# Two streams of 64-row matmuls in place of 128-row ones, and activations kept in SBUF

## The reference

```
w   = softmax of weight_gen over its 7 taps
x1  = for each token and each of 8 heads of 24 features: sum over the 7 last tokens of w[tap] * x
h1  = x1 @ moe_w_in        (192 -> 2048);   g1 = maximum(0.01 * h1, h1)
x2  = g1 @ moe_w_out       (2048 -> 192)
h2  = x2 @ moe2_w_in       (192 -> 2048);   g2 = where(h2 > 0, h2, exp(minimum(h2, 0)) - 1)
out = g2 @ moe2_w_out      (2048 -> 192)
```

## Time and profile before

| | us |
|---|---|
| median of 3 runs | 1212.63 (1212.58 to 1213.23) |
| profiled execution | 1211.23 |
| its span in the trace | 1209.4 |
| TensorE matmuls busy | 1185.8 (98%) |
| VectorE busy | 814.8 (67%) |
| ScalarE busy | 746.2 (62%) |
| GpSimd busy | 355.1 (29%) |

### The profile page before, as it was taken

The page is one execution under the profiler, slowest core; times in us unless marked ns, Lnnn a source line. Parts: engine busy times, 40 slices in busy tenths (PEclk is TensorE's granted clock), DMA queues, the critical chain, the costliest instruction groups (busy, mean ns, idle before and its releaser), DMA issues.

```text
span 1209.4 us, 14562 instructions
## 1 busy us (share of the span) xinstructions
PE 1185.8 (98%) x5208; PEld 973.0 (80%) x5208; DVE 814.8 (67%) x778; ACT 746.2 (62%) x815; POOL 355.1 (29%) x216
## 2 busy tenths in 40 slices
PE   7798999999999999999999999999999999999998
PEld 5586888888888888888888888888888888888887
DVE  7877775766767666675766767666676766766555
ACT  3365757666575665757666575665756656575675
POOL 5725060240704206061250704307061250700000
PEclk9999999999999999999999999999999999999999
DMA  7231112011110211112010110211112010100001
GB/s 194 61 98 37 27 40 64 26 49 26 51 51 26 66 35 49 26 39 62 26 49 26 47 54 26 63 39 49 26 39 62 26 49 26 39 26 27 14 17 36
DMA packets 44642, 54.24 MB, mean 45 GB/s; under 512 B 4116, under 2 KB 32914, under 8 KB 44624
## 3 DMA queue, kind: packets, MB, share of 16 engines
q1 hardware_dynamic: 44624, 54.01, 14.7%
HBM read 36.29 MB, written 17.69 MB: 45 GB/s over the span
## 4 chain that ended last, share of the span: by engine, by line
PE 92%; DVE 5%; ACT 1%; DMA 0%; POOL 0%; issue 0%; SPq 0%; POOLq 0%; ACTq 0%
PE hidden L516 46%; PE y_b L545 9%; PE y_b L546 9%; PE y_a L552 9%; PE y_a L551 9%; PE y_a L550 9%; DVE hid_lo L952 1%; DVE hidden L913 1%; ACT hid_hi L810 1%; DVE up_b_lo L832 1%; DVE up_a_lo L832 1%; DMA xw<-in_x_dram 0%; PE turn L585 0%; DVE dn L345 0%; PE turn L589 0%; DVE dn L344 0%
## 5 line engine op out<-in xcount | busy, mean ns | idle before, releaser
L952 DVE TENSOR_TENSOR hid_lo<-hidden,hid_hi 128x1024 fp32r<-128x1024 f32 x254 | 311.0, 1225 | 242.0 <-ACT hid_hi L810 242.0
L810 ACT ACTIVATE hid_hi<-hidden 128x1024 fp32r<-128x1024 f32 x254 | 260.8, 1027 | 329.3 <-DVE hidden L913 200.8
L284 POOL TENSOR_TENSOR mix<-xw,wk 128x768 f32<-128x768 f32 x15 | 23.3, 1554 | 684.8 <-DVE wk L859 681.8
L916 DVE SCALAR_TENSOR_TENSOR hidden<-act,hidden 128x1024 f32<-128x1024 f32 x129 | 157.5, 1221 | 98.7 <-ACT act L785 96.7
L516 PE MATMUL hidden<-in_a_hi,up_a_hi 128*128 128x512 f32 x510 | 200.8, 394 | 12.2 <-DVE hid_lo L952 11.6
L545 PE MATMUL y_b<-hid_hi,dn 128*128 128x512 f32 x512 | 199.5, 390 | 1.2 <-DVE dn L345 1.2
L546 PE MATMUL y_b<-hid_lo,dn 128*128 128x512 f32 x512 | 199.3, 389 | 0.0
L552 PE MATMUL y_a<-hid_lo,dn 128*128 128x512 f32 x512 | 199.2, 389 | 0.0
L550 PE MATMUL y_a<-hid_hi,dn 128*128 128x512 f32 x512 | 199.2, 389 | 0.0
L551 PE MATMUL y_a<-hid_hi,dn 128*128 128x512 f32 x512 | 199.2, 389 | 0.0
L516 PE MATMUL hidden<-in_b,up_b_lo 128*128 128x512 f32 x510 | 199.0, 390 | 0.0
(11 more groups left out here) (100 smaller groups left out, 1140.9 us busy)
## 6 DMA issues: line engine op xcount, KB each, us to landing
xw<-in_x_dram SPq DMA_DIRECT2D x14, 960.0 KB
raw_b<-squares_out SPq DMA_DIRECT2D x60, 96.0 KB, 2.2
out_dram<-staged SPq DMA_DIRECT2D x15, 384.0 KB, 2.4
squares_in<-prod SPq DMA_DIRECT2D x56, 96.0 KB, 2.0
squares_out<-ya SPq DMA_DIRECT2D x15, 256.0 KB, 2.0
raw_a<-squares_in SPq DMA_DIRECT2D x14, 256.0 KB, 2.8
raw_d<-in_moe_w_out_dram SPq DMA_DIRECT2D x8, 384.0 KB, 6.2
raw_a<-in_moe_w_in_dram SPq DMA_DIRECT2D x8, 256.0 KB, 4.9
```

The source lines that it names most:

```text
L284: ops.tensor_tensor(dst, src, w, ALU.mult).then_inc(done, 1)
L810: nc.scalar.activation(hid_hi[:, s % 2, :], hidden[:, s % 2, :], ACT.Copy).then_inc(s_hi, 1)
L916: nc.vector.scalar_tensor_tensor(out=h, in0=a, scalar=-1.0, in1=h, op0=ALU.add, op1=ALU.max).then_inc(done, 1)
L952: nc.vector.tensor_tensor(hid_lo[:, s % 2, :], h, hid_hi[:, s % 2, :].bitcast(f32), ALU.subtract).then_inc(s_lo, 1)
```

## The change

Every steady matmul is cut to 64 of the 128 rows: one works on partitions 0 to 63 (LOW), the next on 64 to 127 (HIGH), and they alternate, each stream with its own PSUM bank at a time. What filled 64 of 128 rows twice is now packed closer: `up_b_lo` holds only the lower half of its columns on each half of the rows, and `up_pair` does both halves of a step in one pair, with a second copy of the input `in_b_up` on the upper rows. So a step has 19 pairs in place of 20 matmuls. `y_a` has two banks, one for each stream, which are added at the end (`add_y`). `up` is split into a first and a second half, and `down` into `down_open` and `down_close`; each half of `up` fills one bank from the LOW rows and the other from the HIGH rows, and the second half crosses over.

The nonlinearity writes into `act` in SBUF instead of `hidden`, and `hid_hi` and `hid_lo` read it there. So the first half of `up` waits for the nonlinearity of two steps before (`s_g`), and `down_open` for its `hid_lo`. `take_y` and `add_y` move ahead of the step's own work in step 1. In step 1, `down_close` stands ahead of the second half of `up`.

```diff
         def up(m, src, g, s, second):
+                if not second:
+                    for n in range(3):
+                        up_a(LOW, 0, n)
+                        up_a(HIGH, 1, n)
+                    up_b(LOW, 0)
+                    up_b(HIGH, 1)
+                    up_pair(m, src, s)[1].then_inc(s_open, 1)
+                    return
+                pe.wait_ge(s_open, g)
+                for n in range(3):
+                    up_a(LOW, 1, n)
+                    up_a(HIGH, 0, n)
+                half1 = up_b(LOW, 1, stop=True)
+                half0 = up_b(HIGH, 0, stop=True)
...
+            def up_pair(m, src, s, stop=False):
+                cols = slice(s * P, (s + 1) * P)
+                low = nc.tensor.matmul(hidden[:, s % 2, HALF[0]], up_b_lo[m][LOW, cols], in_b[src][LOW, :], start=False, stop=stop)
+                high = nc.tensor.matmul(hidden[:, s % 2, HALF[1]], up_b_lo[m][HIGH, cols], in_b_up[src][HIGH, :], start=False, stop=stop)
+                return low, high
...
+            def down_close(m, s, d):
+                down_a(m, s, LOW, 0, 1)
+                down_a(m, s, HIGH, 1, 2)
+                down_a(m, s, LOW, 0, 2)
+                pe.wait_ge(s_yblow, d + 1)
+                down_b(m, s, HIGH, 0, 0)
+                down_a(m, s, LOW, 1, 0)
...
             def phase(m, c, ph, dm, dc):
-                        pe.wait_ge(s_lo, g - 1)
-                    up(m, input_of(m, c), g, s)
+                        pe.wait_ge(s_g, g - 1)
+                    up(m, input_of(m, c), g, s, False)
...
+                    pe.wait_ge(s_lo, g - 1)
+                    of, step = (dm, ST - 2 + s) if s < 2 else (m, s - 2)
+                    down_open(of, step, g - 2, ph if s == 2 and dm is not None else None)
+                    if s == 1:
+                        down_close(of, step, g - 2)
+                        up(m, input_of(m, c), g, s, True)
                     else:
+                        up(m, input_of(m, c), g, s, True)
+                        down_close(of, step, g - 2)
...
# ScalarE
+                    nc.scalar.activation(in_b_up[input_of(1, c)][D2:P, :], yb[0][:, :], ACT.Copy)
                     nc.scalar.activation(in_b[input_of(1, c)][0:D2, :], yb[0][:, :], ACT.Copy).then_inc(s_mhi, 1)
...
+                    if s == 1 and dm is not None:
+                        take_y(dm, dc, ph - 1)
                     act_e.wait_ge(s_up, g + 1)
-                        act_e.wait_ge(s_g, g - 1)
+                        act_e.wait_ge(s_lo, g - 1)
-                    if s == 1 and dm is not None:
-                        take_y(dm, dc, ph - 1)
...
-                    nc.scalar.activation(hid_hi[:, s % 2, :], hidden[:, s % 2, :], ACT.Copy).then_inc(s_hi, 1)
+                    nc.scalar.activation(hid_hi[:, s % 2, :], act[:, s % 2, :], ACT.Copy).then_inc(s_hi, 1)
# VectorE
-                    nc.vector.tensor_tensor(h, h, a, ALU.max).then_inc(done, 1)
+                    nc.vector.tensor_tensor(a, h, a, ALU.max).then_inc(done, 1)
...
-                    nc.vector.tensor_tensor(hid_lo[:, s % 2, :], h, hid_hi[:, s % 2, :].bitcast(f32), ALU.subtract).then_inc(s_lo, 1)
+                    nc.vector.tensor_tensor(hid_lo[:, s % 2, :], act[:, s % 2, :], hid_hi[:, s % 2, :].bitcast(f32), ALU.subtract).then_inc(s_lo, 1)
```

More of the change, by code:

```diff
@@ L548, in down_a @@
[L548 to L559, removed]
+                low, high = up_pair(0, input_of(0, 0), 0, stop=True)
@@ new lines, in up_first, with down_b, down_a @@
+                low.then_inc(s_up1, 1)
+                high.then_inc(s_up, 1)
+            def down_b(m, s, rows, i, n):
+                f = 2 * s + i
+                v = (hid_hi, hid_lo)[n]
+                start, stop = f == 0 and n == 0 and rows == LOW, f == FT - 1 and n == 1 and rows == HIGH
+                return nc.tensor.matmul(y_b[:, :], dn[m][rows, f, P:2 * P], v[rows, s % 2, HALF[i]], start=start, stop=stop)
+            def down_a(m, s, rows, i, n):
+                f = 2 * s + i
+                first, v = ((0, hid_hi), (2 * P, hid_hi), (0, hid_lo))[n]
+                bank = y_a[0] if rows == LOW else y_a[1]
+                return nc.tensor.matmul(bank[:, :], dn[m][rows, f, first:first + P], v[rows, s % 2, HALF[i]],
+                                        start=(f == 0 and n == 0), stop=(f == FT - 1 and n == 2))
@@ L561, in down_last @@
             def down_last():
                 s = ST - 1
[L564 to L570, removed]
-                last.then_inc(s_dn, 1)
+                wait_half(pe, s_lo, s_lo1, END, 0)
@@ L584, in sum_first_mix @@
                     for j in range(J):
-                        last = nc.tensor.matmul(turn_cols[:, 0, j], term[:, j, 0:P], ident[:, :], start=False, stop=(end and j == J - 1))
+                        last = nc.tensor.matmul(by_token(turn_a)[:, j], term[:, j, 0:P], ident[:, :], start=False, stop=(end and j == J - 1))
                     if end:
@@ L588, in sum_first_mix, with transpose_mix @@
                     for j in range(J):
[L589 removed]
+                        last = nc.tensor.matmul(by_token(turn_b)[:, j], term[:, j, P:D], ident[:, :], start=False, stop=(end and j == J - 1))
                     last.then_inc(s_mixt if end else s_termu, 1)
[L592 removed]
+            def transpose_mix(c, part):
                 pe.wait_ge(s_mix, c + 1)
[L596 removed]
+                pe.wait_ge(s_xin, 2 * c + part)
+                first, last_col = (0, P) if part == 0 else (P, D)
                 for j in range(J):
[L598 to L600 removed]
+                    last = nc.tensor.transpose(by_token(transposed(c)[part])[:, j], mix[:, j, first:last_col], ident[:, :])
                 last.then_inc(s_mixt, 1)
```

213 lines of the change are left out of this document (138 added, 75 removed).

## The result

The changed kernel takes 1263.41 us (median, 1260.8 to 1265.63) against 1212.76: ratio 1.0416, interval [1.0398, 1.0433]. It is slower by 50.7 us; the forecast was slower by 28.4. The profiled execution is the slowest of its four (1265.63), so the spans of the two profiles are 54.4 us apart.

A forecast was written before the change was run, and what follows sets the result against it. TensorE, busy 98% of the span, was taken as the bound. A chunk of 74.7 us, +2.0, gave +26 over 13 chunks; start +6 and end -2.5 made +29.5 on 1211.23: 1241 us, range 1196 to 1290.

The forecast's parts named there:

- the likeliest case: Whole kernel: the forecast of 1241 us, own range 1226 to 1262, chance 0.63.
- A pair in one slot: TensorE's steady steps: two 64-row matmuls take one slot of 0.2267 us, so a step is 4.31 us, a chunk 68.9.
- MLP 2, 2.6 a chunk: Shorter distances: stall 0.6 in MLP 2, ScalarE's pace 0.2, 1.8 at the next MLP 1 pass; 2.6 us a chunk.
- Lock, 3.1 a chunk: MLP 1 passes: VectorE's `hid_lo` from SBUF and GpSimd's mixing exclude each other, stalling TensorE 3.1 us a chunk.
- The layout: Hand-laid VectorE and GpSimd timeline of an MLP 1 pass: stalls of 2.8 us at step 5, 0.3 at step 6.
- A chunk of 74.7: Steady chunk: 68.9 + 2.6 + 3.1, with 0.1 more, 74.7 us; +2.0 on 72.66.
- Start, +6 (0 to 12): First 120 us: more `hid_lo` waits (+4) and costs of the first passes add 6 us, range 0 to 12.
- End, -2.5: Last passes: no mixing (-1.8), last two MLP 2 passes -1.0 each, work behind the last matmul +1.3; -2.5 us.
- slow pairs: Rival: a pair takes longer than a slot, 0.248 us giving 1300 us, 0.27 about 1370; chance 0.15.
- The lock does not bite: Rival: `hid_lo` and mixing miss each other, a chunk of 71.6, about 1195 us; chance 0.17.

The follow-up runs named there:

- GpSimd only writing: GpSimd's mixing products and additions of chunks 1 to 15 replaced by instructions that only write: 1194.21 us on the kernel before, 1190.63 on the changed kernel.
- the mended order with activations in SBUF: Changed kernel, activations left in SBUF, with `up`'s second half after two pairs of `down` and `take_y` behind the step's own work: 1249.92 us, ratio 1.0315.

## Why the prediction was right, and where it was short

*Sign, mechanism and places: right.* The time lies in the range, 22 us above the forecast and 1 above the likeliest case's own range. The mechanisms are those that the prediction named; the size of the start was not.

- *A pair in one slot*: right, 0.227.
- *MLP 2, 2.6 a chunk*: measured 0.59 in step 3 and 1.84 at the start of MLP 1's pass, with ScalarE's loop at 4.36. Right to 0.1 each. The copies to `in_b_up` cost nothing, as the row at 612.54 shows. That `ylow` and `ya` ahead of Relu(1) cost nothing agrees with these waits, but was not measured by itself.
- *Lock, 3.1 a chunk*: 0.77 for `hid_lo` of step 4, 0.18, and 1.77 for that of step 5, together 2.7. The layout had put 2.8 on step 5 and 0.3 behind it: step 4 was late already. Size right.
- *A chunk of 74.7*: measured 75.33. Long waits are 5.2 (forecast 5.5), 0.6 more lie in slots of 0.33 behind them (not foreseen), and all that is no wait is 69.5 (69.2). Two of the twelve chunks are 1.5 longer, see the last section. Together 12 x 0.6 + 3 = 10 us over the forecast.
- *Start, +6 (0 to 12)*: this is the term that was mis-sized: +15.2 at the third `ylow`, of which 3 are there when the mixing of chunk 1 starts, at 32.16. Two of those 3 are no work of the change: the first product of the program waits for the arrival of `x` until 10.13 in this profile and until 8.17 in that of before; before's own matmuls with SBUF placement had it at 9.8 as well.

```profile
10.13 2.09 POOL L317 TENSOR_TENSOR prod<-xw,wk 128x192 f32<-128x192 f32 x2 [7.39 <-DMA xw<-in_x_dram]
```

  The step that failed is "idle TensorE, made by VectorE's weight splits beside mixing; there fewer slots help little, five more `hid_lo` wait (+4)". The runs show that the whole of that idle time is the lock (GpSimd only writing takes 16.8 us from before's start), so it was no fixed cost with five waits beside it. Each part of the change makes it longer by itself: the third `ylow` comes 6.5 us later with the SBUF placement alone and 9.1 with pairs and the new order alone, but only 2.6 with all of it and GpSimd only writing on both sides. (Less what the arrival of `x` differs by, these are about 4.8, 8.5 and 2.3, and the 15.2 is 13.2.) So splits and `hid_lo` take turns with mixing instructions, and TensorE, which has no work stored up there and shorter distances than before, passes much of it on; then it works at the lower clock for a few us.
- *End, -2.5*: with one chunk's +2.0 that makes -0.5, measured +4.2. The copy, two additions and transposes behind the last matmul were right: 2.38 us from it to the transposes against 1.14. Missing were the waits of the last steps (1.04 at 1251.66, where no `up` is left for TensorE to work on while `hid_lo` is made) and the wait of 1.74 at the last MLP 1 pass.
- *Slips in the sums*: the sum ends at 1241 for the profiled execution, and the 1.4 us by which the median lies above it were named but not added. The window of the earlier trace rows is 25 to 145, not the first 120 us. Outside 13 chunks of 16 steps lie 48 of the 256 steps, not 56, which takes 1.4 us from the 1300 of "slow pairs". The 0.248 of "slow pairs" is two loads, 220, and twice 14; from the columns it would be 0.241. None of these moves the forecast by more than 1.4 us.

*The rivals.* "The lock does not bite" is excluded by the length of `hid_lo` and by the run without it, which at 1190.6 came near to its 1195. "Slow pairs" is excluded by 0.227. The Trainium skill's rule in *SBUF — State Buffer*, "Who interferes with whom", held in every run: `hid_lo` has means of 1371 to 1452 ns where it reads two SBUF operands beside mixing, and of 1223 to 1225 from PSUM or beside mere writes. Of *TensorE: Matmul & The Clock Gate*, Part 3, the near-simultaneous start of row groups is what the records show, and two groups run at twice the rate here, without the 10% that the rate of four would suggest.

*What the prediction did not see*: it speaks of the SBUF placement as if taking it back would leave only MLP 2's loss. Pairs with activations in PSUM are as slow (1262.1). The new order shortens the distance whichever result is waited for; the SBUF placement bought some of it back and paid with the lock. That the late second half of `up` is the main fault in that order is argued from the distances and from where the waits stand, steps away from `take_y`; it was not run alone.

## What to carry to other kernels

When TensorE's step becomes shorter, write down for each value the way from the matmul that makes it to the one that needs it, in slots, and compare it with what the other engines take; here moving `up`'s second half three pairs forward (eight in step 1), with `take_y` put back, made the difference between 1262 and 1200 us. Before moving a VectorE operand from PSUM to SBUF, look whether GpSimd works on SBUF in the same stretch, above all at the program's start, where nothing is stored up to cover a turn. And replace GpSimd's work by pure writes once: where nobody waits for its results, as here, one run tells what the lock costs the whole kernel.

## What the runs showed of the hardware that was not expected

- Twice in twelve chunks the granted clock fell from 2.4 to 1.2 GHz behind a wait of 1.77 us: the pairs there start 0.427 apart, and the chunk is 1.5 us longer. The same wait in the other ten chunks left it alone, and so did waits of 1.9 us in all twelve chunks of the mended order with activations in SBUF. What sets the two apart was not found.

```profile
271.99 0.53 PE L587 MATMUL y_b<-hid_hi,dn 64*128 64x512 f32 x1 [1.60 <-DVE hid_lo L1074]
...
272.32 0.62 PE L587 MATMUL y_b<-hid_lo,dn 64*128 64x512 f32 x1
...
272.75 0.62 PE L587 MATMUL y_b<-hid_hi,dn 64*128 64x512 f32 x1
```

- TensorE's first slot after a wait is 0.33 instead of 0.227, after each long wait of the steady part where the clock stays up.
- The lock works both ways, and GpSimd pays more than VectorE: it is busy for 74 us more after than before. VectorE loses 96 us to the lock after (882.8 against 786.6 with GpSimd only writing) and 45 before (814.8 against 769.5), so 51 more, of which `hid_lo` has 41 (351.7 against 311.0).
